# Two of four PSUM copies move from ScalarE to VectorE, and the hash dots move from step 11 to step 1 of the next pair

## The chip, the cores and the metric

The kernel runs on one core of one Trainium2 chip. The metric is device time in microseconds (us), lower is better. The kernel before takes 767.3 us, the median of 3 runs (767.23 to 768.35).

## The reference

Sixteen heads of bucketed attention, then two feed-forward layers, in float32:

```python
q_bits = (einsum('bhsd,dk->bhsk', q, proj) > 0)        # 6 bits; k_bits the same
mask = q_bucket[:, :, :, None] == k_bucket[:, :, None, :]
scores = where(mask, scale * q @ k.T, -1e9)
attn = softmax(scores);  attn_out = attn @ v           # B=2, H=8, S=768, D=64
x = attn_out as (1536, 512)
h = x @ w_in;  g = P(h) / (Q(h) + 1e-6);  x = g @ w_out   # d_ff 2048, cubic over quadratic
h = x @ w_in2; out = (h - tanh(h)) @ w_out2
```

## The kernel before, in words

The heads are worked on in 8 pairs, p = 0 to 7. A pair has 12 steps, n = 0 to 11: six tiles of 128 query rows for each of its two heads. Pair 0, pair 6 and pair 7 are written out, pairs 1 to 5 are the passes of a loop on each engine. Every engine has its own list of instructions in a fixed order, and waits on semaphores. In step n:

- TensorE (PE) turns the exponentials of tile n (`pe_tile`, L379: six 128x128 transposes into the two banks `turn_ps[0]` and `turn_ps[1]`), does the aux work of the step, then the scores of tile n+3 (`pe_scores`, L253, into `slot`), then a third of a group of three tiles' product with v (`pe_pv`, L337 and L339, into `pv_ps`).
- ScalarE (ACT) first takes a finished group out of `pv_ps` where one is due (`act_out`, L502, at n = 0, 3 and 6), rounds the turned tile (`pt_hi`, L520, two halves), does the aux work, takes the exponential of tile n+2 (`act_exp`, L459), and at n = 4 and 10 prepares the sums (`act_sum`, L468).
- VectorE (DVE) takes the remainder of the turned tile (`pt_lo`, L613, two halves), at n = 5 and 10 takes the reciprocal of the sums (`dve_scale`, L579, which waits for `act_sum`), does the aux work, and reduces the minimum of tile n+3 (`dve_rowmin`, L571). At n = 9 it takes one group out of `pv_ps` (`dve_out`, L596).

TensorE's transposes of step n+1 wait, half by half, for the `pt_lo` of step n: both halves of `turn_ps` are single buffers.

The aux work prepares q and k of a later pair, through one PSUM bank, `aux_ps`, whose nine uses per pair follow one another strictly:

1. four turns: q and k (x = 0, 1), each in two halves (h = 0, 1), are transposed into `aux_ps` (`pe_turn`, L266) and copied to `turned` (`act_turned`, L405, into `q_t` and `k_t`). For pair p+2 this is in steps 7 to 10 of pair p. A turn waits until the one before has been copied out.
2. the dots with the hash planes (`pe_dots`, L275) and their signs (`dve_bits`, L583), in step 11.
3. four one-hot products (`pe_hot`, L286), the q ones copied out by DVE (`dve_hot_q`, L589), the k ones by ACT (`act_hot_k`, L449), in steps 1 to 4 of the next pair, by the table HOT_STEPS.

Pair 0 prepares pair 1 in the same way in its own first steps: turns in steps 0 and 1 (two in each, one before the scores and one after them), dots in step 2, one-hots in steps 3 to 6.

GpSimd (POOL) splits `q_t` and `k_t` into two parts (`pool_split_qk`), and SyncE (SP) issues the DMAs that copy the parts to their operands. After pair 7 come 96 steps of the two feed-forward layers on the same engines; the change does not touch them.

Of the kernel before, what the change touches and what calls it, by code (L numbers as in the profile page):

```python
# [10 lines left out]
ALU = mybir.AluOpType  # L11
# [7 lines left out]


AUX_USES = 9
AUX_ACT = 6
AUX_DVE = 3

AHEAD = 3
RING = 4
# [1 line left out]
BIAS = 8  # L28


def build(nc, q, k, v, proj, w_in1, w_out1, coef_a, coef_b, w_in2, w_out2,
          identity, patterns, bit_counts, out):
    B, H, S, D = q.shape
# [57 lines left out]
    with top:  # L91
# [91 lines left out]

        HOT_STEPS = {1: (0, 0), 2: (1, 0), 3: (0, 1), 4: (1, 1)}
        G = T // 2
        GROUPS = TILES // G

# [14 lines left out]
        def aux_hot(b, x, h):  # L204
            return BIAS + b * AUX_USES + 5 + 2 * h + x + 1

        def act_turn(b, x, h):
            return BIAS + b * AUX_ACT + 2 * x + h + 1

        def act_hot(b, h):  # L210
            return BIAS + b * AUX_ACT + 4 + h + 1

        def dve_dot(b):
            return BIAS + b * AUX_DVE + 1

        def dve_hot(b, h):
            return BIAS + b * AUX_DVE + 1 + h + 1

        def last_scores(p, e):
            m = e * T + T - 1  # L220
# [36 lines left out]

        def pe_turn(eng, b, x, h):
            if x or h:
                eng.wait_ge(sems["aux_act"], act_turn(b, x, h) - 1)  # L260
            elif not is_zero(b):
                eng.wait_ge(sems["aux_act"], act_hot(b - 1, 1))
            if h == 0:
                eng.wait_ge(loads["qk"[x]], 32 * (b + 1))
            for c in range(T // 2):
                mm = eng.transpose(aux_ps[:, c * P:(c + 1) * P],  # L266
                                   nat[x][:, h * (T // 2) + c, :, :], ident[:, :])
            mm.then_inc(sems["aux"], 1)

        def pe_dots(eng, b):  # L270
            eng.wait_ge(sems["aux_act"], act_turn(b, 1, 1))
            for x in range(2):
                for h in range(2):
                    o = (2 * x + h) * KB
                    mm = eng.matmul(aux_ps[o:o + KB, 0:HALF], proj_bd[:, x, :],  # L275
                                    turned[x][:, h * HALF:(h + 1) * HALF], start=True, stop=True)
            mm.then_inc(sems["aux"], 1)
# [66 lines left out]
        def pe_att(eng, p, first=False, prepare=True, turn=True, last=False):  # L344
            for n in range(TILES - G * last):
                pe_tile(eng, p, n)
                if first and n < 2:
                    pe_turn(eng, 1, n, 0)
                if first and n == 2:
                    pe_dots(eng, 1)  # L350
                if prepare and n - 2 * first in HOT_STEPS:
                    pe_hot(eng, p + 1, *HOT_STEPS[n - 2 * first])
                if turn and 7 <= n < 11:
                    pe_turn(eng, p + 2, (n - 7) // 2, (n - 7) % 2)
                if turn and n == 11:
                    pe_dots(eng, p + 2)
                if first and n + AHEAD == T:
                    eng.wait_ge(loads["t_op1"], 6)
                if n + AHEAD < TILES or not last:
                    pe_scores(eng, p, n + AHEAD)  # L360
                if first and n < 2:
                    pe_turn(eng, 1, n, 1)
                if n >= G:
                    pe_pv(eng, p, n // G - 1, n % G, last)
                elif not first:
                    pe_pv(eng, p - 1, GROUPS - 1, n)
            if last:
                pe_handover(eng, p)
# [77 lines left out]
        def act_hot_k(eng, b, h):  # L446
            eng.wait_ge(sems["aux"], aux_hot(b, 1, h))
            staged_free(eng, b)
            eng.activation(st_hot[1][:, h * HALF:(h + 1) * HALF], aux_ps[:, 0:HALF],  # L449
                           ACT.Relu, bias=counts[:, 1:2]).then_inc(sems["aux_act"], 1)  # L450
# [53 lines left out]
        def act_att(eng, p, first=False, prepare=True, turn=True, last=False):  # L504
            for n in range(TILES):
                N = p * TILES + n
                c, i = divmod(n, G)
                if i == 0 and c >= 2:
                    if last:
                        act_low(eng, c - 2)  # L510
                    else:
                        act_out(eng, p, c - 2)
                elif i == 0 and not first:
                    act_out(eng, p - 1, c + GROUPS - 2)
                for h in range(2):
                    eng.wait_ge(sems["pt"], BIAS + 2 * N + h + 1)
                    if i == 0:
                        eng.wait_ge(sems["pv"], BIAS + GROUPS * p + c - 1)
                    k0 = h * (T // 2)
                    eng.activation(pt_hi[:, c % 2, k0:k0 + T // 2, i * P:(i + 1) * P],  # L520
                                   turn_ps[h][:, 0:HALF].rearrange("r (k n) -> r k n", n=P),
                                   ACT.Copy).then_inc(sems["pt_hi"], 1)
                if first and n < 2:
                    eng.wait_ge(loads["t_op1"], 3 * n + 3)
                    act_turned(eng, 1, n, 0)
                if turn and 7 <= n < 11:
                    act_turned(eng, p + 2, (n - 7) // 2, (n - 7) % 2)
                if n + AHEAD - 1 < TILES or not last:
                    act_exp(eng, p, n + AHEAD - 1)
                if n in (4, 9 if last else 10):  # L530
                    act_sum(eng, p, n // T)
                if first and n < 2:
                    act_turned(eng, 1, n, 1)
                if prepare and HOT_STEPS.get(n - 2 * first, (0, 0))[0] == 1:
                    act_hot_k(eng, p + 1, HOT_STEPS[n - 2 * first][1])
                if last and n == TILES - 3:
                    act_step(eng, 0)
                if last and n == TILES - 2:
                    act_reads(eng, 1)
                    act_low(eng, GROUPS - 2)  # L540
            if last:
                act_step(eng, 1, reads=False)
                act_low(eng, GROUPS - 1)
# [30 lines left out]
        def dve_scale(eng, p, e):  # L574
# [3 lines left out]
                eng.wait_ge(loads[f"scale_out{e}"], 16 * p)  # L578
            eng.reciprocal(row_inv[:, e, :], row_eps[:, e, :]).then_inc(sems["recip"], 1)  # L579

        def dve_bits(eng, b):
            eng.wait_ge(sems["aux"], aux_dot(b))
            eng.tensor_scalar(bits[:, :], aux_ps[:, 0:HALF], 0.0, None, ALU.is_gt  # L583
                              ).then_inc(sems["aux_dve"], 1)
# [13 lines left out]
        def dve_att(eng, p, first=False, prepare=True, turn=True, last=False):  # L598
            for n in range(TILES):
                N = p * TILES + n  # L600
                c, i = divmod(n, G)
                if i == 0 and c >= 2:
                    if last:
                        dve_sum(eng, c - 2)
                    else:
                        dve_out(eng, p, c - 2)
                elif i == 0 and not first:
                    dve_out(eng, p - 1, c + GROUPS - 2)
                for h in range(2):
                    eng.wait_ge(sems["pt_hi"], BIAS + 2 * N + h + 1)  # L610
                    k0 = h * (T // 2)
                    dst = (slice(None), c % 2, slice(k0, k0 + T // 2), slice(i * P, (i + 1) * P))
                    eng.tensor_tensor(pt_lo[dst],  # L613
                                      turn_ps[h][:, 0:HALF].rearrange("r (k n) -> r k n", n=P),
                                      pt_hi[dst].bitcast(F32), ALU.subtract
                                      ).then_inc(sems["pt_lo"], 1)
                if n in (5, 9 if last else 10):
                    dve_scale(eng, p, n // T)
                if last and n == TILES - 3:
                    dve_step(eng, 0)  # L620
                if last and n == TILES - 2:
                    dve_sum(eng, GROUPS - 2)
                if first and n == 2:
                    dve_bits(eng, 1)
                if prepare and HOT_STEPS.get(n - 2 * first, (1, 0))[0] == 0:
                    dve_hot_q(eng, p + 1, HOT_STEPS[n - 2 * first][1])
                if turn and n == 11:
                    dve_bits(eng, p + 2)
                if n + AHEAD < TILES or not last:
                    dve_rowmin(eng, p, n + AHEAD)  # L630
            if last:
                dve_step(eng, 1)
                dve_sum(eng, GROUPS - 1)
# [1 line left out]


        def pool_split_qk(eng, b, x):
            eng.wait_ge(sems["aux_act"], act_turn(b, x, 1))
            staged_free(eng, b)
            eng.sem_inc(loads["pool_here"], 1)  # L640
            eng.tensor_copy(st_hi[x][:, :], turned[x][:, :]).then_inc(sems["hi"], 1)
# [715 lines left out]
```

## Time and profile before

| | before |
|---|---|
| median of 3 runs | 767.3 us |
| the profiled execution | 767.21 us |
| its span | 765.0 us |
| PE busy in the span | 751.2 us (98%) |
| DVE busy | 536.6 us (70%) |
| ACT busy | 478.4 us (63%) |
| POOL busy | 155.5 us (20%) |

The span is from the first to the last instruction; 2.2 us of the profiled execution lie around it. The granted TensorE clock is 1.000 over the whole span. Busy time of TensorE is modelled and overlaps the next matmul, so a short wait between two groups of matmuls does not show as idle time: such waits are read from the distances between the starts of the same instruction in successive steps.

### The profile page before, as it was taken

Reading aid. Unit: us, or ns where it says so; the run is one execution under the profiler, and the core shown is the slowest. Engines: PE = TensorE matmul, PEld = TensorE weight load, DVE = VectorE, ACT = ScalarE, POOL = GpSimd, SP = SyncE. Lnnn points to the kernel's source line nnn. Section 1 sums busy time; section 2 is a strip of 40 time slices with the busy share of each in tenths; the row PEclk is TensorE's granted clock in tenths of the full one; section 3 lists DMA queues with packets and bytes.
Section 4 is the critical chain, followed back from the end, with each engine's and each line's share of the span. In section 5 each row is a group of like instructions: output and inputs, shape, how many; then the busy total and the mean of one; then the engine's idle time right before and its main releaser. Section 6 shows DMA issues by size and latency. Waiting matters only on the chain.

```text
span 765.0 us, 11965 instructions
## 1 busy us (share of the span) xinstructions
PE 751.2 (98%) x3840; PEld 642.1 (84%) x3840; DVE 536.6 (70%) x856; ACT 478.4 (63%) x940; POOL 155.5 (20%) x133
## 2 busy tenths in 40 slices
PE   5999999999999999999999999999999999999998
PEld 3899999999998877888888888888888888888886
DVE  4888988988997999999988898955442322233222
ACT  5989988988997877788766876755332222222221
POOL 5784665566566000000000000000000000000000
PEclk9999999999999999999999999999999999999999
DMA  7678778877753410000000233330000100001001
GB/s 196 145 170 204 172 178 185 188 177 179 164 130 99 146 51 32 1 1 1 0 1 15 55 95 99 93 87 1 0 1 1 56 0 1 0 1 56 0 1 56
DMA packets 65243, 58.11 MB, mean 76 GB/s; under 512 B 31792, under 2 KB 50480, under 8 KB 65200
## 3 DMA queue, kind: packets, MB, share of 16 engines
q1 hardware_dynamic: 63488, 57.09, 29.6%
q10 hardware_dynamic: 1712, 0.46, 0.3%
q8 instruction: 25, 0.41, 0.2%
q14 instruction: 18, 0.15, 0.1%
HBM read 29.57 MB, written 3.19 MB: 43 GB/s over the span
## 4 chain that ended last, share of the span: by engine, by line
PE 84%; DVE 12%; issue 2%; ACT 1%; ACTq 0%; DVEq 0%
PE acc L822 28%; PE h_ps L793 27%; PE slot L253 9%; PE turn_ps L379 8%; PE pv_ps L337 4%; PE pv_ps L339 4%; DVE sqr L967 2%; DVE pol L988 2%; DVE pol L999 2%; DVE pol L974 1%; DVE pol L980 1%; PE aux_ps L266 1%; DVE sqr L991 1%; DVE wout_lo L1028 1%; DVE g_lo L1012 1%
## 5 line engine op out<-in xcount | busy, mean ns | idle before, releaser
L793 PE MATMUL h_ps<-x_hi,win_lo 128*128 128x512 f32 x384 | 149.7, 390 | 0.0
L793 PE MATMUL h_ps<-x_lo,win_hi 128*128 128x512 f32 x384 | 149.4, 389 | 0.0
L793 PE MATMUL h_ps<-x_hi,win_hi 128*128 128x512 f32 x384 | 149.4, 389 | 0.0
L843 ACT ACTIVATE g_hi<-pol 128x512 fp32r<-128x512 f32 x96 | 60.8, 633 | 125.6 <-PE acc L822 100.4
L1012 DVE TENSOR_TENSOR g_lo<-pol,g_hi 128x512 fp32r<-128x512 f32 x96 | 66.0, 687 | 97.9 <-ACT g_hi L843 97.7
L613 DVE TENSOR_TENSOR pt_lo<-turn_ps,pt_hi 128x384 fp32r<-128x384 f32 x192 | 97.8, 550 | 18.8 <-ACT pt_hi L520 17.3
L520 ACT ACTIVATE pt_hi<-turn_ps 128x384 fp32r<-128x384 f32 x192 | 84.1, 494 | 15.2 <-PE turn_ps L379 13.8
L571 DVE TENSOR_REDUCE row_min<-slot 128x1 f32<-128x768 f32 x96 | 90.4, 942 | 1.5 <-PE slot L253 1.5
L459 ACT ACTIVATE E<-slot,row_min 128x768 f32<-128x768 f32 x96 | 88.1, 918 | 4.2 <-DVE row_min L571 2.6
L793 PEld LDWEIGHTS h_ps<-x_lo,win_hi 128*128 128x128 f32 x384 | 72.1, 188 | 15.0
L793 PEld LDWEIGHTS h_ps<-x_hi,win_hi 128*128 128x128 f32 x384 | 72.1, 188 | 15.0
L793 PEld LDWEIGHTS h_ps<-x_hi,win_lo 128*128 128x128 f32 x384 | 72.0, 188 | 14.7
L1006 DVE TENSOR_TENSOR pol<-h_ps,mag 128x512 f32<-128x512 f32 x48 | 33.1, 691 | 67.7 <-ACT mag L866 67.2
L379 PE MATMUL turn_ps<-ident,E 128*128 128x128 f32 x576 | 79.6, 273 | 0.0
L866 ACT ACTIVATE mag<-h_ps 128x512 f32<-128x512 f32 x48 | 28.7, 598 | 78.4 <-PE h_ps L793 75.2
L822 PE MATMUL acc<-g_hi,wout_lo 128*128 128x512 f32 x192 | 75.2, 392 | 1.0 <-DVE g_lo L1012 0.8
L822 PE MATMUL acc<-g_hi,wout_hi 128*128 128x512 f32 x192 | 74.7, 389 | 0.0
L822 PE MATMUL acc<-g_lo,wout_hi 128*128 128x512 f32 x192 | 74.7, 389 | 0.0
L822 PE MATMUL acc<-wout_lo,g_hi 128*128 128x512 f32 x192 | 74.7, 389 | 0.0
L822 PE MATMUL acc<-wout_hi,g_hi 128*128 128x512 f32 x192 | 74.7, 389 | 0.0
L822 PE MATMUL acc<-wout_hi,g_lo 128*128 128x512 f32 x192 | 74.7, 389 | 0.0
L379 PEld LDWEIGHTS turn_ps<-ident,E 128*128 128x128 f32 x576 | 68.0, 140 | 5.3 <-DVE pt_lo L613 1.9
(119 smaller groups left out, 1375.6 us busy)
## 6 DMA issues: line engine op xcount, KB each, us to landing
win_raw<-in_moe_w_in SPq DMA_DIRECT2D x32, 256.0 KB, 3.2
wout_raw<-in_moe_w_out SPq DMA_DIRECT2D x32, 256.0 KB, 3.0
q_nat<-in_q SPq DMA_DIRECT2D x16, 192.0 KB, 3.3
v_nat<-in_v SPq DMA_DIRECT2D x8, 384.0 KB, 3.4
scale<-softmax_scale SPq DMA_DIRECT2D x16, 192.0 KB, 3.2
k_nat<-in_k SPq DMA_DIRECT2D x14, 192.0 KB, 3.6
qA<-q_hi SPq DMA_DIRECT2D x14, 192.0 KB, 2.6
qB<-q_hi SPq DMA_DIRECT2D x14, 192.0 KB, 3.0
```

The source lines that it names most:

```text
L253: mm = eng.matmul(slot[m % 2][:, h, 0:HALF], ops[e][0][:, i * P:(i + 1) * P], ops[e][1][:, h * HALF:(h + 1) * HALF], start=first, stop=not ...
L337: eng.matmul(pv_ps[:, 0:HALF], vv, pt_hi[:, c % 2, kt, :], start=kt == 0, stop=False)
L379: mm = eng.transpose(turn_ps[h][:, c3 * P:(c3 + 1) * P], E[:, n % RING, kt * P:(kt + 1) * P], ident[:, :])
L459: eng.activation(halves(E[:, m % RING, :]), slot[m % 2][:, :, 0:HALF], ACT.Exp, bias=row_min[:, m % RING:m % RING + 1], scale=-1.0, accum_ ...
L520: eng.activation(pt_hi[:, c % 2, k0:k0 + T // 2, i * P:(i + 1) * P], turn_ps[h][:, 0:HALF].rearrange("r (k n) -> r k n", n=P), ACT.Copy).t ...
L571: eng.tensor_reduce(row_min[:, m % RING:m % RING + 1], slot[m % 2][:, :, 0:HALF], AX.XY, ALU.min).then_inc(sems["rowmin"], 1)
L613: eng.tensor_tensor(pt_lo[dst], turn_ps[h][:, 0:HALF].rearrange("r (k n) -> r k n", n=P), pt_hi[dst].bitcast(F32), ALU.subtract).then_inc( ...
L793: mm = eng.matmul(h_ps[t % 4][:, :], w[:, ws], columns(x, kt, c), start=kt + n == 0, stop=kt == KT - 1 and n == 2)
L822: mm = eng.matmul(acc[i][:, :], l, r if layer else r[:, :], start=j + n == 0, stop=j == J - 1 and n == 2)
L843: eng.activation(g_hi[:, t % TEMPS, :], pol[:, t % TEMPS, :], ACT.Copy).then_inc(mlp_sems["g_hi"], 1)
L1006: eng.tensor_tensor(pol[:, t % TEMPS, :], h_ps[t % 4][:, :], mag[:, t % 2, :], ALU.subtract).then_inc(mlp_sems["g"], 1)
L1012: eng.tensor_tensor(g_lo[:, b, :], pol[:, b, :], g_hi[:, b, :].bitcast(F32), ALU.subtract).then_inc(mlp_sems["g_lo"], 1)
```

## The change

The dots and the bits of a pair are no longer made in step 11 of the pair before the one that uses them to prepare, but in step 1 of that next pair; the four one-hots then follow in steps 2 to 5 in place of 1 to 4. In pair 0 dots and one-hots stay where they are (steps 2, and 3 to 6). Of the four copies out of `aux_ps` after the turns, VectorE takes the first (q, half 0) and the last (k, half 1), with a `tensor_scalar`; ScalarE keeps the two between. In the loop these are steps 7 and 10 for VectorE, 8 and 9 for ScalarE. In pair 0 VectorE takes its first copy in step 0 behind its `pt_lo`, and its second in step 1 behind its `rowmin`. All that counts on these semaphores follows.

```diff
-AUX_ACT = 6
-AUX_DVE = 3
+AUX_ACT = 4
+AUX_DVE = 5
-        HOT_STEPS = {1: (0, 0), 2: (1, 0), 3: (0, 1), 4: (1, 1)}
+        DOT_STEP = 1
+        HOT_STEPS = {2: (0, 0), 3: (1, 0), 4: (0, 1), 5: (1, 1)}
+        def turn_out(b, x, h):
+            if x == h:
+                return sems["aux_dve"], BIAS + b * AUX_DVE + x + 1
+            return sems["aux_act"], BIAS + b * AUX_ACT + x + 1
...
         def pe_turn(eng, b, x, h):
             if x or h:
-                eng.wait_ge(sems["aux_act"], act_turn(b, x, h) - 1)
+                done, count = turn_out(b, *divmod(2 * x + h - 1, 2))
+                eng.wait_ge(done, count)
...
         def pe_dots(eng, b):
-            eng.wait_ge(sems["aux_act"], act_turn(b, 1, 1))
+            done, count = turn_out(b, 1, 1)
+            eng.wait_ge(done, count)
... (pe_att)
-                if prepare and n - 2 * first in HOT_STEPS:
-                    pe_hot(eng, p + 1, *HOT_STEPS[n - 2 * first])
+                if prepare and not first and n == DOT_STEP:
+                    pe_dots(eng, p + 1)
+                if prepare and n - first in HOT_STEPS:
+                    pe_hot(eng, p + 1, *HOT_STEPS[n - first])
                 if turn and 7 <= n < 11:
                     pe_turn(eng, p + 2, (n - 7) // 2, (n - 7) % 2)
-                if turn and n == 11:
-                    pe_dots(eng, p + 2)
... (act_att)
-                if first and n < 2:
+                if first and n == 1:
                     eng.wait_ge(loads["t_op1"], 3 * n + 3)
-                    act_turned(eng, 1, n, 0)
-                if turn and 7 <= n < 11:
+                    act_turned(eng, 1, 1, 0)
+                if turn and n in (8, 9):
                     act_turned(eng, p + 2, (n - 7) // 2, (n - 7) % 2)
...
-                if first and n < 2:
-                    act_turned(eng, 1, n, 1)
-                if prepare and HOT_STEPS.get(n - 2 * first, (0, 0))[0] == 1:
-                    act_hot_k(eng, p + 1, HOT_STEPS[n - 2 * first][1])
+                if first and n == 0:
+                    eng.wait_ge(loads["t_op1"], 3 * n + 3)
+                    act_turned(eng, 1, 0, 1)
+                if prepare and HOT_STEPS.get(n - first, (0, 0))[0] == 1:
+                    act_hot_k(eng, p + 1, HOT_STEPS[n - first][1])
... (new)
+        def dve_turned(eng, b, x, h):
+            eng.wait_ge(sems["aux"], aux_turn(b, x, h))
+            eng.wait_ge(sems["lo"], BIAS + 2 * b + x - 1)
+            eng.tensor_scalar(turned[x][:, h * HALF:(h + 1) * HALF], aux_ps[:, 0:HALF],
+                              -1.0 / float(D) ** 0.5 if x == 0 else 1.0, None, ALU.mult
+                              ).then_inc(sems["aux_dve"], 1)
... (dve_att)
-                if prepare and HOT_STEPS.get(n - 2 * first, (1, 0))[0] == 0:
-                    dve_hot_q(eng, p + 1, HOT_STEPS[n - 2 * first][1])
-                if turn and n == 11:
-                    dve_bits(eng, p + 2)
+                if prepare and not first and n == DOT_STEP:
+                    dve_bits(eng, p + 1)
+                if prepare and HOT_STEPS.get(n - first, (1, 0))[0] == 0:
+                    dve_hot_q(eng, p + 1, HOT_STEPS[n - first][1])
+                if first and n == 0:
+                    eng.wait_ge(loads["t_op1"], 3)
+                    dve_turned(eng, 1, 0, 0)
+                if turn and n in (7, 10):
+                    dve_turned(eng, p + 2, (n - 7) // 2, (n - 7) % 2)
                 if n + AHEAD < TILES or not last:
                     dve_rowmin(eng, p, n + AHEAD)
+                if first and n == 1:
+                    eng.wait_ge(loads["t_op1"], 6)
+                    dve_turned(eng, 1, 1, 1)
```

`pool_split_qk` waits for both copies of its operand, one on each engine's semaphore.

VectorE in steps 10 and 11 of pair 0; L579 is the reciprocal of the sums, L583 the bits. Before:

```order
L613 TENSOR_TENSOR pt_lo<-turn_ps,pt_hi 128x3x128 x2
L579 RECIPROCAL row_inv<-row_eps 128x6
L571 TENSOR_REDUCE row_min<-slot 128x1
L613 TENSOR_TENSOR pt_lo<-turn_ps,pt_hi 128x3x128 x2
L583 TENSOR_SCALAR bits<-aux_ps 128x384
L571 TENSOR_REDUCE row_min<-slot 128x1
```

The same place in the changed kernel (its lines are numbered higher):

```order
L627 TENSOR_TENSOR pt_lo<-turn_ps,pt_hi 128x3x128 x2
L586 RECIPROCAL row_inv<-row_eps 128x6
L591 TENSOR_SCALAR k_t<-aux_ps 128x384
L578 TENSOR_REDUCE row_min<-slot 128x1
L627 TENSOR_TENSOR pt_lo<-turn_ps,pt_hi 128x3x128 x2
L578 TENSOR_REDUCE row_min<-slot 128x1
```

The copy of the last turn stands between the reciprocal and the minimum of step 10; the bits of step 11 are gone from it.

ScalarE from step 2 to the start of step 6, shown in pair 6, which is written out and has the same steps as the loop there; L449 is the copy of a k one-hot, L502 the copy out of `pv_ps`, L468 the sums. Before:

```order
L459 ACTIVATE E,row_sum<-slot,row_min 128x768
L449 ACTIVATE k_hot<-aux_ps,counts 128x384
L502 ACTIVATE x_raw<-pv_ps 128x384
L520 ACTIVATE pt_hi<-turn_ps 128x3x128 x2
L459 ACTIVATE E,row_sum<-slot,row_min 128x768
L520 ACTIVATE pt_hi<-turn_ps 128x3x128 x2
L459 ACTIVATE E,row_sum<-slot,row_min 128x768
L468 ACTIVATE row_eps<-row_sum,sum_eps 128x6
L449 ACTIVATE k_hot<-aux_ps,counts 128x384
L520 ACTIVATE pt_hi<-turn_ps 128x3x128 x2
L459 ACTIVATE E,row_sum<-slot,row_min 128x768
L502 ACTIVATE x_raw<-pv_ps 128x384
```

The same place in the changed kernel:

```order
L465 ACTIVATE E,row_sum<-slot,row_min 128x768
L508 ACTIVATE x_raw<-pv_ps 128x384
L526 ACTIVATE pt_hi<-turn_ps 128x3x128 x2
L465 ACTIVATE E,row_sum<-slot,row_min 128x768
L455 ACTIVATE k_hot<-aux_ps,counts 128x384
L526 ACTIVATE pt_hi<-turn_ps 128x3x128 x2
L465 ACTIVATE E,row_sum<-slot,row_min 128x768
L474 ACTIVATE row_eps<-row_sum,sum_eps 128x6
L526 ACTIVATE pt_hi<-turn_ps 128x3x128 x2
L465 ACTIVATE E,row_sum<-slot,row_min 128x768
L455 ACTIVATE k_hot<-aux_ps,counts 128x384
L508 ACTIVATE x_raw<-pv_ps 128x384
```

The first k one-hot has moved behind the `x_raw` of step 3, the second from behind the sums of step 4 to just ahead of the `x_raw` of step 6.

VectorE at the start of pair 0, steps 0 to 2. Before:

```order
L613 TENSOR_TENSOR pt_lo<-turn_ps,pt_hi 128x3x128 x2
L571 TENSOR_REDUCE row_min<-slot 128x1
L613 TENSOR_TENSOR pt_lo<-turn_ps,pt_hi 128x3x128 x2
L571 TENSOR_REDUCE row_min<-slot 128x1
L613 TENSOR_TENSOR pt_lo<-turn_ps,pt_hi 128x3x128 x2
```

In the changed kernel:

```order
L627 TENSOR_TENSOR pt_lo<-turn_ps,pt_hi 128x3x128 x2
L591 TENSOR_SCALAR q_t<-aux_ps 128x384
L578 TENSOR_REDUCE row_min<-slot 128x1
L627 TENSOR_TENSOR pt_lo<-turn_ps,pt_hi 128x3x128 x2
L578 TENSOR_REDUCE row_min<-slot 128x1
L591 TENSOR_SCALAR k_t<-aux_ps 128x384
L627 TENSOR_TENSOR pt_lo<-turn_ps,pt_hi 128x3x128 x2
```

The copy of the first turn stands behind the two `pt_lo` of step 0, that of the last turn behind the minimum of step 1.

## Rows read from the trace of the kernel before

**Rows 1.** The page, part 4: shares of the chain that ended last, by engine

```profile
PE 84%; DVE 12%; issue 2%; ACT 1%; ACTq 0%; DVEq 0%
```

**Rows 2.** Timeline of PE, pair 3: start us, duration us, engine, line, operation

```profile
102.12 0.82 PE L379 MATMUL turn_ps<-ident,E 128*128 128x128 f32 x6
104.17 0.82 PE L379 MATMUL turn_ps<-ident,E 128*128 128x128 f32 x6
...
108.58 0.82 PE L379 MATMUL turn_ps<-ident,E 128*128 128x128 f32 x6
...
110.94 0.82 PE L379 MATMUL turn_ps<-ident,E 128*128 128x128 f32 x6
...
113.17 0.82 PE L379 MATMUL turn_ps<-ident,E 128*128 128x128 f32 x6
...
115.29 1.01 PE L379 MATMUL turn_ps<-ident,E 128*128 128x128 f32 x6
...
117.53 0.82 PE L379 MATMUL turn_ps<-ident,E 128*128 128x128 f32 x6
...
127.08 0.82 PE L379 MATMUL turn_ps<-ident,E 128*128 128x128 f32 x6
...
130.13 0.81 PE L379 MATMUL turn_ps<-ident,E 128*128 128x128 f32 x6
```

**Rows 3.** Timeline of TensorE's weight loads in pair 3, step 6

```profile
115.28 0.31 PEld L379 LDWEIGHTS turn_ps<-ident,E 128*128 128x128 f32 x3 [0.23 <-DVE pt_lo L613]
```

**Rows 4.** Timeline of ACT in pair 3

```profile
102.40 0.49 ACT L502 ACTIVATE x_raw<-pv_ps 128x384 f32<-128x384 f32 x1 [0.70 <-PE pv_ps L339]
102.79 0.87 ACT L520 ACTIVATE pt_hi<-turn_ps 128x384 fp32r<-128x384 f32 x2
103.53 0.92 ACT L459 ACTIVATE E<-slot,row_min 128x768 f32<-128x768 f32 x1
...
107.74 0.91 ACT L459 ACTIVATE E<-slot,row_min 128x768 f32<-128x768 f32 x1
...
108.64 0.57 ACT L449 ACTIVATE k_hot<-aux_ps,counts 128x384 fp32r<-128x384 f32 x1
109.10 0.49 ACT L502 ACTIVATE x_raw<-pv_ps 128x384 f32<-128x384 f32 x1
...
125.99 0.50 ACT L405 ACTIVATE k_t<-aux_ps 128x384 f32<-128x384 f32 x1
126.36 0.92 ACT L459 ACTIVATE E<-slot,row_min 128x768 f32<-128x768 f32 x1
```

**Rows 5.** Timeline of DVE in pair 3

```profile
114.67 1.02 DVE L613 TENSOR_TENSOR pt_lo<-turn_ps,pt_hi 128x384 fp32r<-128x384 f32 x2 [0.47 <-ACT pt_hi L520]
...
127.58 0.19 DVE L579 RECIPROCAL row_inv<-row_eps 128x6 f32<-128x6 f32 x1 [0.81 <-ACT row_eps L468]
127.69 0.92 DVE L571 TENSOR_REDUCE row_min<-slot 128x1 f32<-128x768 f32 x1
128.52 1.01 DVE L613 TENSOR_TENSOR pt_lo<-turn_ps,pt_hi 128x384 fp32r<-128x384 f32 x2
129.45 0.55 DVE L583 TENSOR_SCALAR bits<-aux_ps 128x384 bf16<-128x384 f32 x1
129.91 0.95 DVE L571 TENSOR_REDUCE row_min<-slot 128x1 f32<-128x768 f32 x1
131.31 1.02 DVE L613 TENSOR_TENSOR pt_lo<-turn_ps,pt_hi 128x384 fp32r<-128x384 f32 x2 [0.45 <-ACT pt_hi L520]
```

**Rows 6.** Timeline of DVE and weight loads in pair 0, steps 0 to 2

```profile
18.38 1.01 DVE L613 TENSOR_TENSOR pt_lo<-turn_ps,pt_hi 128x384 fp32r<-128x384 f32 x2
...
19.14 0.31 PEld L266 LDWEIGHTS aux_ps<-ident,q_nat 128*128 128x128 f32 x3 [0.30 <-ACT q_t L405]
...
21.70 0.95 DVE L571 TENSOR_REDUCE row_min<-slot 128x1 f32<-128x768 f32 x1
22.84 0.11 PEld L275 LDWEIGHTS aux_ps<-q_t,proj_bd 128*32 128x32 f32 x2 [0.30 <-ACT k_t L405]
```

More of the change, by code:

```diff
@@ L205, in aux_hot @@
             return BIAS + b * AUX_USES + 5 + 2 * h + x + 1
-        def act_turn(b, x, h):
-            return BIAS + b * AUX_ACT + 2 * x + h + 1
+        def turn_out(b, x, h):
+            if x == h:
+                return sems["aux_dve"], BIAS + b * AUX_DVE + x + 1
+            return sems["aux_act"], BIAS + b * AUX_ACT + x + 1
         def act_hot(b, h):
-            return BIAS + b * AUX_ACT + 4 + h + 1
+            return BIAS + b * AUX_ACT + 2 + h + 1
         def dve_dot(b):
-            return BIAS + b * AUX_DVE + 1
+            return BIAS + b * AUX_DVE + 2 + 1
         def dve_hot(b, h):
-            return BIAS + b * AUX_DVE + 1 + h + 1
+            return BIAS + b * AUX_DVE + 3 + h + 1
         def last_scores(p, e):
@@ L637, in pool_split_qk @@
         def pool_split_qk(eng, b, x):
-            eng.wait_ge(sems["aux_act"], act_turn(b, x, 1))
+            for h in range(2):
+                done, count = turn_out(b, x, h)
+                eng.wait_ge(done, count)
             staged_free(eng, b)
```

## The prediction

> **What bounds the kernel now.** I read the page first. The chain that ended last is TensorE for 84% and VectorE for 12% [rows 1], and the granted clock is full throughout, so clock is no term. The attention part, which alone is changed, ends before the feed-forward steps begin, and what it gains or loses shifts the rest unchanged. Inside a pair I then laid the starts of TensorE's turn (L379) side by side [rows 2]. Call Sn the start of step n. A step without aux work takes 2.05 us (102.12 to 104.17). Pair 3 runs from 102.12 to 130.13, 28.01 us. Nearly all of it is TensorE working without pause; a change of order can only act on the few waits, and I find two:
>
> - Step 3 takes 2.36 (108.58 to 110.94), step 4 with the same work 2.23 (110.94 to 113.17). The 0.13 more is the third one-hot waiting for ScalarE's first `k_hot`, which starts only at 108.64, 0.06 after S3 [rows 4].
> - Steps 5 and 6 hold no aux work and take 2.12 and 2.24, together 0.26 more than 2 x 2.05. The weight loads name the cause: TensorE waits for `pt_lo` [rows 3]. That `pt_lo` started at 114.67 [rows 5], 0.55 before the moment at which step 6 could have begun (113.17 + 2.05 = 115.22), and it was late since ScalarE had the sums and the second `k_hot` ahead of its `pt_hi`. I use this pair of numbers as a gauge: a `pt_lo` that starts 0.55 before TensorE wants its next turn costs 0.26, each 0.1 less lead 0.1 more, and none from a lead of about 0.81.
>
> So 0.39 us per pair is all that order could win in the five pairs of the loop, about 2 us of 767.
>
> **The change part by part.** TensorE keeps every instruction. The dots step is the longest (127.08 to 130.13, 3.05 us, so the dots cost 1.00 with what they hold up), and that 1.00 is paid in step 1 instead of step 11. In itself this is nothing. But in step 11 it was also time in which VectorE and ScalarE caught up with TensorE. That cover is what I look at.
>
> *The seam between pairs.* Step 10 on VectorE sits idle 0.81 for ScalarE's sums and then does the reciprocal at 127.58 and the minimum at 127.69 [rows 5]. ScalarE loses its `k_t` copy there, so its exponential starts 0.37 earlier (125.99 instead of 126.36 [rows 4]), the sums and the reciprocal too: 127.21. The new `k_t` copy on VectorE is queued behind the reciprocal, at 127.32 (0.11 later, as the minimum was). Its price is that of the bits, the nearest row: 0.46 from its start to that of the next (129.45 to 129.91 [rows 5]). The minimum then starts at 127.78, and `pt_lo` of step 11 0.83 behind it (127.69 to 128.52) at 128.61 in place of 128.52. So far nothing is lost. But TensorE has no dots in step 11 and wants its next turn at 127.08 + 2.05 = 129.13, not at 130.13. The lead is 0.52, by the gauge a wait of 0.29. It comes at six seams, pair 0 to 1 up to pair 5 to 6: 6 x 0.29 = +1.74. It is bounded below by 0, if VectorE gets through 0.29 earlier, and above by what the price of a copy can be: the `k_hot`-like 0.57 instead of 0.46 gives 0.40 a seam, +2.4.
>
> *The first k one-hot.* It is now behind the `x_raw` of step 3. `x_raw` starts 0.28 after the step's turn (102.12 to 102.40), `pt_hi` 0.39 later, the exponential 0.74 later, and `k_hot` 0.90 behind the exponential (107.74 to 108.64 [rows 4]): S3 + 2.31, which is 0.08 after S4 = S3 + 2.23. Before it was 0.06 after S3. So the wait of 0.13 goes from step 3 and stands in step 4, some 0.03 longer: 5 x 0.03 = +0.15. Bounds: -0.13 and +0.1 each.
>
> *The second k one-hot.* Step 4 of ScalarE is relieved, and the wait of 0.26 at S6 goes. But now `k_hot` of step 5 stands just ahead of the `x_raw` of step 6. `x_raw` follows `k_hot` by 0.46 (108.64 to 109.10 [rows 4]); if `k_hot` lies as it did in step 2, it starts 0.06 after S6, `x_raw` 0.52 after; if ScalarE is a little ahead, having no q one-hot before its minimum, 0.41. From `x_raw` to `pt_lo` it is 0.90 (the seam: turn 130.13, `x_raw` 0.28 later, `pt_lo` 131.31 [rows 2, 5]). `pt_lo` of step 6 thus starts 1.31 to 1.42 after S6, and TensorE wants step 7 at 2.05: leads of 0.74 to 0.63, waits of 0.07 to 0.18. I take 0.12, so 5 x (0.12 - 0.26) = -0.70, bounds -1.3 and 0.
>
> *The q copy in step 7.* VectorE takes 0.46 more in a step of 2.40 with two `pt_lo` (1.02) and a minimum (0.95): 2.4 in all, and step 8 leaves it time. Its aux bank is needed again only a step later. Zero, hidden by TensorE's extra transposes in steps 7 to 10; at worst 0.1 a pair.
>
> *The start, pair 0.* Here turns come two to a step, and TensorE waits for each copy before the next: the load at 19.14 stood waiting for ScalarE's `q_t`, that at 22.84 for `k_t` [rows 6]. Now the first copy is behind VectorE's two `pt_lo`, which start at 18.38; 0.93 later (128.52 to 129.45 [rows 5]) the copy starts at 19.31. Release comes 0.61 after a start of this size (`pt_lo` 114.67, load 115.28 [rows 3, 5]): 19.92 instead of 19.14, +0.78. The next turns and the scores of tile 4 follow about 0.75 later, so the minimum moves from 21.70 to 22.45. The last copy stands behind that minimum, 0.94 later at 23.39, and the dots get it at 24.00 in place of 22.84: +1.16, which I round to +1.15. Nothing of it is hidden, since TensorE's own work fills the steps that follow. Bounds 0.8 to 1.5.
>
> POOL, SP: their instructions keep their order. POOL's splits of the loop start when the DMAs of the old operands land, not when the copies end, and the one-hot DMAs are issued behind other DMAs later than step 5. No term.
>
> Sum: 1.15 + 1.74 + 0.15 - 0.70 = +2.3 us. On the profiled execution, 767.21 (765.0 span and 2.2 around it), this is 769.5; the median of before lies 0.1 higher, so 769.6.
>
> A rule of the Trainium skill speaks against the copies themselves. Here the nearest row has VectorE's read of 384 columns out of the bank at 0.55 (the bits) and ScalarE's at 0.50 (`k_t`) [rows 4, 5]. "Advanced Engine Details and Errata", section "The Read-Write Bubble", says that ScalarE is closer to PSUM and VectorE closer to SBUF, to be used accordingly. By that rule the two moved copies cost 0.05 each more, the trace agrees, but as the sum above shows it is the place in the queue, not this 0.05, that sets the time.
>
> **The rivals.**
>
> *Not slower: the seam holds.* If `pt_lo` of step 11 starts by 128.32, a lead of 0.81, no seam costs anything, and if ScalarE is far enough ahead at S6 and S3 both old waits go: 5 x -0.39 = -1.95, against +1.15 at the start: 766.5. For it speaks VectorE's idle 0.81 in step 10, which any earlier sum would turn into lead. Against it: the sum can only move by the 0.37 that the copy gives back, and the copy's 0.46 is laid on top. Clearly faster than before only if the start also loses less than I say.
>
> *The loop's turn-around is exposed.* At the seam each engine goes through the end of its loop. VectorE has 0.45 idle there, ScalarE 0.70 [rows 4, 5], which today would hide it. In the new order I leave VectorE nearly none. If all of the 0.45 were needed, the start of `pt_lo` in step 0 would slip by that and 0.4 be lost in each of five passes: +2.0 more, 771.6. For it: the idle time comes back in every pair. Against it: both idle times are put down to data, `pt_hi` and `pv_ps`, not to the branch. The Trainium skill ("Advanced Engine Details and Errata", section "Control Flow Timing") gives a compare-and-branch about 108 ns; no row here shows it alone, and by that figure the loss would be some 0.1 a pass, 770.1.
>
> *Milder.* The gauge is too strict, and seam and step 7 cost half of what I take while the start costs 0.9: about 768.1, within the error of no change.
>
> **How the numbers follow.** My forecast, 769.6, with its own range 768.7 to 770.6: 0.5. Milder, 768.1: 0.2. Exposed turn-around, 771.6: 0.15. The seam holds, 766.5: 0.15, a part of it below 765.8. Within 0.2% is what a measurement can't tell from no change, 765.8 to 768.8. The forecast and the turn-around give slower 0.60 (a little of the forecast's low end is not over the bound), the milder case and most of the last give same 0.29, and 0.11 is left for faster. Range 766.8 to 771.8.
>
> **What would show it.** Right: the first dots near 24.0 us in the trace and TensorE about 1.1 us late from pair 0, step 3, on; step 11 and the step after it together some 0.3 over 4.10, with weight loads idle for `pt_lo`; step 3 without its 0.13 and step 4 with it; steps 5 and 6 at 4.10 and step 7 about 0.1 longer; a loop pair near 28.1. Wrong: a loop pair at 27.7 or below (the seam holds), at 28.4 or above with idle on VectorE or ScalarE that no data explains (the turn-around), or the first dots before 23.3.

## The result, and the profile after

| | before | after |
|---|---|---|
| median | 768.79 us (767.13 to 770.22, 21 runs) | 770.18 us (768.88 to 771.26, 21 runs) |
| profiled execution, its span | 767.21, 765.0 us | 771.07, 769.2 us |

The changed kernel is slower: ratio 1.002, interval 1.0012 to 1.0029. The forecast was 769.6 from a median of 767.3, that is +2.3 us; measured are +1.4 us, and the median is inside the range. The median of the kernel before is itself 1.5 us above the 767.3 of its first three runs. The 4.2 us between the two profiled spans must not be taken for the effect: about 2 us of it is something else, which comes last in this section.

First a loop pair, by the starts of TensorE's turn. This is the timeline of PE in the changed kernel, pair 3 from step 0 on and the first two steps of pair 4, columns as in [rows 2]:

```profile
104.74 1.01 PE L385 MATMUL turn_ps<-ident,E 128*128 128x128 f32 x6
...
112.23 0.81 PE L385 MATMUL turn_ps<-ident,E 128*128 128x128 f32 x6
...
114.44 0.82 PE L385 MATMUL turn_ps<-ident,E 128*128 128x128 f32 x6
...
116.69 0.81 PE L385 MATMUL turn_ps<-ident,E 128*128 128x128 f32 x6
...
118.90 0.82 PE L385 MATMUL turn_ps<-ident,E 128*128 128x128 f32 x6
...
120.94 0.95 PE L385 MATMUL turn_ps<-ident,E 128*128 128x128 f32 x6
...
123.45 0.82 PE L385 MATMUL turn_ps<-ident,E 128*128 128x128 f32 x6
...
130.62 0.82 PE L385 MATMUL turn_ps<-ident,E 128*128 128x128 f32 x6
...
132.85 1.01 PE L385 MATMUL turn_ps<-ident,E 128*128 128x128 f32 x6
...
135.10 0.82 PE L385 MATMUL turn_ps<-ident,E 128*128 128x128 f32 x6
```

The pair takes 28.11 (104.74 to 132.85), the mean over the five loop pairs is 28.16 against 28.01 before. Step 3 is 2.21, step 4 2.25, step 6 2.04: the two old waits, in step 3 and in steps 5 and 6 [rows 2], are gone or nearly so. Step 7 is 2.51 instead of 2.40. The new wait is at the seam: step 11 takes 2.23 and step 0 2.25, together 0.38 over 2 x 2.05.

VectorE on its way to the seam, to be held against [rows 5], and the weight loads that wait for it, as in [rows 3]:

```profile
129.27 1.02 DVE L627 TENSOR_TENSOR pt_lo<-turn_ps,pt_hi 128x384 fp32r<-128x384 f32 x2 [0.41 <-ACT pt_hi L526]
130.72 0.19 DVE L586 RECIPROCAL row_inv<-row_eps 128x6 f32<-128x6 f32 x1 [0.43 <-ACT row_eps L474]
130.91 0.56 DVE L591 TENSOR_SCALAR k_t<-aux_ps 128x384 f32<-128x384 f32 x1
131.38 0.95 DVE L578 TENSOR_REDUCE row_min<-slot 128x1 f32<-128x768 f32 x1
132.25 1.01 DVE L627 TENSOR_TENSOR pt_lo<-turn_ps,pt_hi 128x384 fp32r<-128x384 f32 x2
```

```profile
132.85 0.31 PEld L385 LDWEIGHTS turn_ps<-ident,E 128*128 128x128 f32 x3 [0.32 <-DVE pt_lo L627]
133.31 0.31 PEld L385 LDWEIGHTS turn_ps<-ident,E 128*128 128x128 f32 x3 [0.16 <-DVE pt_lo L627]
```

The idle time before the reciprocal has shrunk from 0.81 to 0.43 since ScalarE is relieved, and then the copy spends more than was won. TensorE wanted its turn at 130.62 + 2.05 = 132.67, and `pt_lo` of step 11 started 0.42 before that.

What disturbs the comparison is the start. TensorE's weight loads between 11 and 23 us, of the changed kernel in its profiled execution:

```profile
11.40 0.10 PEld L317 LDWEIGHTS aux_ps<-bits,pats 128*128 128x128 bf16 x1 [2.03 <-issue]
11.44 0.11 PEld L317 LDWEIGHTS turn_ps<-bits,pats 128*128 128x128 bf16 x1
11.71 0.15 PEld L317 LDWEIGHTS pv_ps<-bits,pats 128*128 128x128 bf16 x1 [0.17 <-issue]
...
14.19 0.65 PEld L257 LDWEIGHTS slot<-kB,qB 128*128 128x128 f32 x2
...
18.66 1.40 PEld L385 LDWEIGHTS turn_ps<-ident,E 128*128 128x128 f32 x6
...
22.38 0.69 PEld L385 LDWEIGHTS turn_ps<-ident,E 128*128 128x128 f32 x6
```

and of the kernel before, in the same order of the program:

```profile
13.63 0.36 PEld L253 LDWEIGHTS slot<-kB,qB 128*128 128x128 f32 x2
...
17.13 0.75 PEld L379 LDWEIGHTS turn_ps<-ident,E 128*128 128x128 f32 x6
```

The same two loads take 0.65 in the one and 0.36 in the other, the same six 1.40 and 0.75. TensorE ran at about half its pace from 11.7 to 21 us, after 2.03 us without a load; the granted clock is listed as 1.00 in both. But the profiles of two of the experiments show the same pace with the clock beside it. From 15 to 20 us, first in the changed kernel, then in the run with the start alone put back (busy time and count of PE, PEld, DVE, ACT, POOL, then the granted clock, DMA share, GB/s):

```profile
15.00:20.00 5.00, 4.07 (x15) 3.49 (x14) 2.70 (x3) 2.22 (x6) 4.60 (x4) 1.00 0.58 181
15.00:20.00 5.00, 4.06 (x15) 3.49 (x14) 2.71 (x4) 2.20 (x6) 4.71 (x5) 0.50 0.71 223
```

The same 15 and 14 instructions take the same time, and the second row lists a clock of 0.50, the lower of TensorE's two levels (1.2 GHz of 2.4). In that run it reads 0.50 from 15 to 21 us, and in the run with the copies alone moved, where the six loads again take 1.40, from 14 to 21. So the clock was most likely at the lower level in the changed kernel too, and its profile does not list it.

The instructions up to there are the same in both kernels. Step 0 of pair 0 starts at 18.98 instead of 17.31. The experiments show that this differs from execution to execution, for either kernel.

### The profile page after: what moved, and what is told of

It is laid out like the page before. It is cut to its first block, busy times and chain, and to the rows that moved or that the text cites. A ratio compares the mean times of both kernels' runs of the same rounds, so it can differ in the third digit from the quotient of the medians.

```text
span 769.2 us, 11975 instructions
## 1 busy us (share of the span) xinstructions
PE 756.4 (98%) x3840; PEld 644.9 (84%) x3840; DVE 544.7 (71%) x870; ACT 473.1 (62%) x926; POOL 155.8 (20%) x133
## 4 chain that ended last, share of the span: by engine, by line
PE 84%; DVE 12%; issue 2%; ACT 1%; DMA 1%; SPq 0%; DVEq 0%; ACTq 0%
PE acc L846 28%; PE h_ps L817 27%; PE slot L257 9%; PE turn_ps L385 8%; PE pv_ps L343 4%; PE pv_ps L345 4%; DVE sqr L991 2%; DVE pol L1012 2%; DVE pol L1023 2%; DVE pol L998 1%; DVE pol L1004 1%; PE aux_ps L271 1%; DVE sqr L1015 1%; DVE wout_lo L1052 1%; DVE g_lo L1036 1%
```

## The experiments

Each run was timed beside the kernel before on the same chip. All ratios are against it. Two medians from different comparisons should not be subtracted, as that of the kernel before was 768.79 in the first, 767.76 for the next four runs and 767.52 for the last four.

**The start alone put back.** ScalarE makes pair 1's copies as before, the loop is that of the change:

```diff
-                if first and n == 0:
-                    eng.wait_ge(loads["t_op1"], 3)
-                    dve_turned(eng, 1, 0, 0)
-                if first and n == 1:
-                    eng.wait_ge(loads["t_op1"], 6)
-                    dve_turned(eng, 1, 1, 1)
... (act_att)
+                if first and n < 2:
...
+                    act_turned(eng, 1, n, 0)
...
+                if first and n < 2:
+                    act_turned(eng, 1, n, 1)
```

> The change, but in pair 0 (steps 0 and 1) ScalarE makes all four copies of pair 1's turns, as before; the loop is that of the change. Theory (waits add up: start and seam): the start gives back its 1.15 us, so about 1.1 us below the change and 0.3 above before; a loop pair stays at 28.16 us. Rival (the start costs nothing, the difference lies in the loop and in how early TensorE runs at its full pace): the time of the change, 1.4 us above before.

Median 767.92 us (767.51 to 770.63, 12 runs), ratio 1.0006 (0.9994 to 1.0018). The loop pairs stay at 28.17 in the mean. By the ratios most of the loss is gone with the two copies of pair 0, although the loop still has its seam wait. The rival's 1.4 us above the kernel before lies just at the end of the interval, so the times alone do not rule it out. The profiles do: in both, step 0 of pair 0 starts at the same time and at the slow pace (19.00 here, 18.98 in the change), and steps 0 to 2 take 8.06 here and 8.66 there. So the two copies cost 0.60 at the slow pace; what they cost at full pace is shown further down.

**The dots alone moved.** All copies stay on ScalarE; `DOT_STEP = 1` and the HOT_STEPS of the change:

```diff
-        HOT_STEPS = {1: (0, 0), 2: (1, 0), 3: (0, 1), 4: (1, 1)}
+        DOT_STEP = 1
+        HOT_STEPS = {2: (0, 0), 3: (1, 0), 4: (0, 1), 5: (1, 1)}
```

> The kernel before with dots and one-hots moved as in the change, all copies still on ScalarE. Theory (the seam wait comes from the dots' cover being gone, whoever copies): pt_lo of step 11 starts where it did, 0.61 us before TensorE wants its turn, so 0.20 us wait at the seam by the gauge, 0.04 in step 4, 0.1 in step 7: a loop pair of 27.95, whole time 0.3 below before. Rival (the seam wait is VectorE's extra copy): no seam wait, a loop pair of 27.75, 1.3 below before.

Median 767.43 us (766.57 to 769.86, 12 runs), ratio 1.0002 (0.999 to 1.0014). A loop pair takes 27.93 to 27.95, the last of the five 28.02, with steps 11 and 0 together 4.27 to 4.29, a seam wait of 0.18, and step 7 at 2.51. So the seam wait exists without any copy on VectorE, half as large: it comes from the dots being gone. The rival's 27.75 is out. Steps 3 to 7 are those of the change (2.21, 2.25, 2.21, 2.05, 2.51), so it is the move of dots and one-hots that removed the two old waits.

**The copies alone moved.** The change with dots and one-hots back in step 11 and steps 1 to 4:

```diff
-                if prepare and not first and n == DOT_STEP:
-                    pe_dots(eng, p + 1)
...
+                if turn and n == 11:
+                    pe_dots(eng, p + 2)
... (HOT_STEPS, and the bits and the copies of the one-hots, likewise)
```

> The change with dots and one-hots put back where they were before (step 11, steps 1 to 4): only the two copies are on VectorE. Theory: with the dots in step 11 there is no seam wait, a loop pair is 28.0 as before, and only the start costs: 1.1 us above before. Rival (VectorE has no room for two copies a pair): a loop pair of 28.2 or more, 2 us and more above before.

Median 769.43 us (768.55 to 771.66, 12 runs), ratio 1.0021 (1.0008 to 1.0033). A loop pair takes 28.17 to 28.19, not 28.0: here my expectation failed, and the rival's number (28.2) is met, but not for its reason. All steps are as before except step 11, which takes 3.20 to 3.23 instead of 3.05. The weight load of the dots names what it waits for:

```profile
130.69 0.11 PEld L280 LDWEIGHTS aux_ps<-q_t,proj_bd 128*32 128x32 f32 x2 [0.35 <-DVE k_t L590]
```

The copy of `k_t` sits behind the reciprocal on VectorE and is late for the dots of step 11. So each half of the change has its price at the seam: with the dots in step 11 they wait for the copy, with the dots moved TensorE waits for the `pt_lo` behind the copy. Alone they cost 0.18 and 0.16 a pair, together 0.38.

**The copy ahead of the reciprocal.** The change, with one instruction moved:

```diff
+                if turn and n == 10:
+                    dve_turned(eng, p + 2, 1, 1)
                 if n in (5, 9 if last else 10):
                     dve_scale(eng, p, n // T)
...
-                if turn and n in (7, 10):
-                    dve_turned(eng, p + 2, (n - 7) // 2, (n - 7) % 2)
+                if turn and n == 7:
+                    dve_turned(eng, p + 2, 0, 0)
```

> The change with VectorE's copy of step 10 ahead of the reciprocal instead of behind it. Theory (the seam wait is the chain sums, reciprocal, copy, minimum, pt_lo of step 11): the copy falls into VectorE's idle time before the sums, pt_lo of step 11 starts 0.5 to 0.6 us earlier, its lead is about 1.0, and no seam wait is left: a loop pair of 27.8, 2.0 to 2.3 us below the change. Rival (the loop's turn-around at the seam): the 0.38 us at the seam stay, a loop pair of 28.1, the time of the change.

Median 767.78 us (766.53 to 768.92, 12 runs), ratio 0.9992 (0.9981 to 1.0003). The change has 1.002, so this is some 2.1 us less, and so are the spans of the two profiles (767.1 and 769.2), which start alike, step 0 at 18.99 and 18.98. Loop pairs take 27.77 to 27.79, steps 11 and 0 together 4.11 to 4.12. VectorE at the seam:

```profile
128.26 1.02 DVE L627 TENSOR_TENSOR pt_lo<-turn_ps,pt_hi 128x384 fp32r<-128x384 f32 x2 [0.41 <-ACT pt_hi L526]
129.20 0.55 DVE L591 TENSOR_SCALAR k_t<-aux_ps 128x384 f32<-128x384 f32 x1
129.71 0.19 DVE L586 RECIPROCAL row_inv<-row_eps 128x6 f32<-128x6 f32 x1
129.82 0.92 DVE L578 TENSOR_REDUCE row_min<-slot 128x1 f32<-128x768 f32 x1
130.66 1.02 DVE L627 TENSOR_TENSOR pt_lo<-turn_ps,pt_hi 128x384 fp32r<-128x384 f32 x2
```

The copy fills the gap in which VectorE waited for the sums, the reciprocal has no wait left, and `pt_lo` starts 1.00 before TensorE's next turn (131.68 less 0.02 of wait), where it was 0.42. So with the copies on VectorE the order in its queue decides the seam wait. Compared with the dots alone moved, where the wait was 0.18, even that is gone: ScalarE without its `k_t` copy has the sums 0.37 earlier (2.16 behind S10, there 2.53). Placed so, the two copies on VectorE are worth 0.16 a pair (27.78 against 27.94). The loop's turn-around, one of the rivals, costs nothing visible: it is still there, and of the wait 0.02 at most is left.

**Both mends together.** The two edits above in one kernel:

```diff
-                    dve_turned(eng, 1, 0, 0)
...
-                    dve_turned(eng, 1, 1, 1)
... (and the copy of step 10 ahead of dve_scale)
```

> The change with both mends: ScalarE makes all four copies in pair 0, and VectorE's copy of step 10 stands ahead of the reciprocal. Theory (start and seam are two separate costs): a loop pair of 27.78, the start as before; against before 5 x -0.23 from the loop pairs and nothing else, 1.2 to 1.5 us below before. Rival (they overlap): no more than 0.6 below, as with the seam mended alone.

Median 767.12 us (765.34 to 768.97, 12 runs), ratio 0.9987 (0.9974 to 1.0). Loop pairs 27.76 to 27.79, steps 0 to 2 of pair 0 as before (2.22, 2.44, 2.46). By the trace the gain is there; the spread of 3.6 us between its runs hides it. The time alone does not tell theory from rival: it is 0.4 us below by the medians and 1.0 by the ratio. The last three runs take the spread away.

**TensorE kept busy at the start, on the kernel before.** Extra products into banks that are free, on operands that nobody needs; nothing of the computation is left out:

```diff
         def pe_first(eng):
+            eng.wait_ge(loads["ready"], 4)
+            for _ in range(10):
+                eng.matmul(pv_ps[:, 0:HALF], bits[:, 0:P], bits[:, :], start=True, stop=True)
...
             eng.wait_ge(loads["consts"], 32)
+            for _ in range(4):
+                eng.matmul(slot[1][:, 0, 0:HALF], pats[:, 0, :], pats[:, 0:3, :],
+                           start=True, stop=True)
... (5 more behind the one-hots, 6 more into aux_ps ahead of the third scores;
     VectorE clears bits ahead of them)
```

> The kernel before with 25 extra TensorE products whose results nobody reads, put into its idle time at the start: 10 before the first inputs arrive, 4 behind the first dots, 5 behind the first one-hots, 6 ahead of the third scores. Theory (the scatter of 2 us between runs of one kernel is TensorE falling back to half its pace at about 12 us in some runs, because it is idle there): the weight loads of the start are at full pace in every run, and all runs lie within 1 us, at 767 or, with the first transposes at full pace too, 766. Rival (the scatter comes from the DMAs or from outside): the runs still spread over 3 us with a median near 768.

Median 767.32 us (766.94 to 767.9, 12 runs), ratio 0.9991 (0.9982 to 1.0001). In the same comparison 11 of the 35 runs of the kernel before were above 768.5 us; of these 12 none. The mean granted clock was 0.993 to 0.998 in 8 of the 11 and listed as 1.00 in the other 3; with the products it is 0.999 or 1.00 in all 12. The weight loads of the start, columns as above:

```profile
11.74 0.75 PEld L319 LDWEIGHTS slot<-pats 128*128 128x128 bf16 x5
13.19 0.30 PEld L253 LDWEIGHTS slot<-kA,qA 128*128 128x128 f32 x2 [0.70 <-issue]
13.47 0.36 PEld L253 LDWEIGHTS slot<-kB,qB 128*128 128x128 f32 x2
```

The spread is 1.0 us instead of 3.4, so most of the scatter was TensorE's pace at the start. The hope for 766 was not met: in this execution the first transposes before 7 us ran as slowly as before (three loads in 0.50), in spite of the ten products ahead of them.

**The same products in the changed kernel.** The edit is the one above.

> The change with the same 25 extra products at the start. Theory: with TensorE at full pace in both, it is slower than the kernel before with those products by the cost of start and seams alone: start 1.15, six seams of 0.38, less 5 x 0.24 for the other waits, together 2.2 us; the first dots 1.15 us later than there. Rival (the measured difference was mostly the pace of the start): 1 us or less.

Median 769.1 us (768.22 to 770.2, 12 runs), ratio 1.0015 (1.0005 to 1.0024), and 1.78 us above the kernel before with the same products. Now the start can be compared at one pace. Weight loads of the turns and the dots in pair 0, first here, then in the kernel before with the products:

```profile
19.93 0.31 PEld L271 LDWEIGHTS aux_ps<-ident,q_nat 128*128 128x128 f32 x3 [1.08 <-DVE q_t L602]
...
23.87 0.11 PEld L281 LDWEIGHTS aux_ps<-q_t,proj_bd 128*32 128x32 f32 x2 [0.62 <-DVE k_t L602]
```

```profile
18.92 0.31 PEld L266 LDWEIGHTS aux_ps<-ident,q_nat 128*128 128x128 f32 x3 [0.31 <-ACT q_t L416]
...
22.62 0.11 PEld L275 LDWEIGHTS aux_ps<-q_t,proj_bd 128*32 128x32 f32 x2 [0.30 <-ACT k_t L416]
```

TensorE waits 1.08 for VectorE's first copy where it waited 0.31, and 0.62 for its last where it waited 0.30. Steps 0 to 2 of pair 0 take 8.16 against 7.13: the start costs 1.03. The first dots come 1.25 later, of which 0.23 is there before step 0 (17.32 against 17.09). The theory's 2.2 us is nearer than the rival's 1, but too high. In this one profile TensorE's weight loads also paused for 1.38 in step 9 of pair 6, ahead of the first scores of pair 7, and the matmul names a DMA:

```profile
209.31 0.59 PE L257 MATMUL slot<-kA,qA 128*128 128x384 f32 x2 [1.17 <-DMA kA<-k_hot]
```

It is the slowest of its 12 runs; step 9 took 3.49 here, 2.43 in the run before this, 2.67 in the next and 2.28 in the kernel before. Part of the scatter that is left may be made there, by the DMAs that bring pair 7's operands; I did not test it.

**Everything.** Both mends and the products:

```diff
... (the edits of the two kernels above)
```

> Both mends of the change and the 25 extra products. Theory: the gains add, 1.2 to 1.5 us below the kernel before with the products, and the runs within 1 us of each other; 765 us. Rival: without the scatter nothing is left of the gain.

Median 766.09 us (765.52 to 767.08, 12 runs), ratio 0.9976 (0.9965 to 0.9987). It is 1.23 us below the kernel before with the products and 3.0 below the change with them: faster than both kernels, clear of the error. The rival, that nothing is left, is out. The hoped-for 765 us and a spread within 1 us were missed: the runs lie 1.6 apart.

## Why the prediction was right, point by point

*The direction and the place* were right: slower, by the start and the seam, both through VectorE's queue order and neither through the duration of a copy. VectorE's copy takes 0.55 to 0.56 and ScalarE's 0.50, as read off the nearest rows. That the level of 770.18 came so near to the forecast of 769.6 is in part luck: both kernels ran slower than in the three runs that the forecast started from, through TensorE's pace at the start. "Clock is no term" held for the one profile that was read, not for the other executions.

*The start*: +1.15 predicted, 1.03 measured at full pace, and 0.60 where TensorE is slow anyway. The first dots, forecast near 24.0, come at 23.87 at full pace and at 26.05 in the change's own profile.

*The seam*: 0.29 predicted, 0.38 in the loop's pairs and 0.28 from pair 0 to 1. The gauge held: a lead of 0.42 should cost 0.39. What was off is the lead, 0.42 for 0.52. The reciprocal came where it was forecast (130.72 is S10 + 2.50; 127.21 was S10 + 2.51), but the `k_t` copy 0.19 behind it, not 0.11, and `pt_lo` 0.87 behind the minimum, not 0.83. That moving the dots uncovers the seam is shown by the run with the dots alone, and the part of the copy by the run with the swap.

*The first k one-hot*: this term failed, in sign. I expected the 0.13 to return in step 4 as 0.16; step 4 has 0.04 (2.25 against 2.21). Over both steps a pair gains 0.13, the very bound that I had stated, so the term is -0.65 and not +0.15. `k_hot` was just where I put it, 0.05 after S4:

```profile
114.49 0.57 ACT L455 ACTIVATE k_hot<-aux_ps,counts 128x384 fp32r<-128x384 f32 x1
```

and the one-hot's load came 0.62 after it, as before. But the next weight load followed at once instead of 0.18 later. Before:

```profile
109.26 0.10 PEld L286 LDWEIGHTS aux_ps<-bits,pats 128*128 128x128 bf16 x1
109.44 0.30 PEld L253 LDWEIGHTS slot<-kA,qA 128*128 128x128 f32 x2
```

After:

```profile
115.11 0.10 PEld L292 LDWEIGHTS aux_ps<-bits,pats 128*128 128x128 bf16 x1
115.12 0.36 PEld L257 LDWEIGHTS slot<-kA,qA 128*128 128x128 f32 x2
```

So a lateness of the same size was hidden once and not the other time. Why the load behind follows in one case and not in the other stays open. One difference is in the code: the scores of step 3 are the first of the second head and wait for its operands as well, those of step 4 do not. No run tests this.

*The second k one-hot*: 0.26 to 0.12 predicted. Steps 5 and 6 are free of waits (2.21 with a one-hot, 2.04) and step 7 has 0.11. Right.

*The sum*: in the prediction's terms 1.03 at the start, 0.28 + 5 x 0.38 = 2.18 at the seams, -0.65 and 5 x (0.11 - 0.26) = -0.75 for the one-hots, together 1.81, against 1.78 between the medians at equal pace and 2.3 predicted. The seams were 0.44 too low and the first one-hot 0.80 too high; these two misses partly cancel, which is luck. Counted by pairs it is 1.94: pair 0 takes 0.13 more (28.89 against 28.76 with the products, as step 11 has lost its dots), the loop 5 x 0.15, and pair 6, which now has dots, 1.06 (26.75 against 25.69). The 1.4 between the plain medians has the scatter of the start in it, and the two copies cost less where the start is slow. The rivals: the turn-around costs nothing, the seam does not hold by itself. The milder case, 768.1 or +0.8 us, is out: the seam cost more than I took, not half.

## What to carry to other kernels

Before work is moved off a step, ask which engines used that step to catch up: 1.00 us of TensorE work moved by two steps cost nothing itself but uncovered a wait of 0.18 behind a chain of sums, reciprocal, minimum and remainder on two other engines. An extra instruction whose input is ready belongs ahead of the one that waits, not behind it: the same copy in the idle gap instead of after the reciprocal turned +0.15 a pair into -0.23. And one profile of each kernel can differ for reasons outside the change: compare distances between like instructions, step by step, before the spans.

## What the hardware showed that I had not expected

TensorE can fall to about half its pace for 6 to 9 us at the start (two loads in 0.65 instead of 0.36, until about 21 us), in some executions of one and the same program and not in others. The fall came at 11.7 us in the profile of the change, at 14 and at 15 in the two that list a granted clock of 0.50 for it. Stretches of 1.5 to 2.2 us without a weight load came before it, but the kernel before has such stretches too (1.89, 1.51 and 1.81) and did not fall in its profile. The clock column does not always show the fall: it read 1.00 over one such stretch and 0.50 over another with the same loads at the same pace. Like loads held side by side show it each time. Nearly a third of the runs of the kernel before (11 of 35) lay above 768.5 us, and with TensorE given something to do in those stretches none of 12 did.
